# One of four low parts moves from GpSimd to VectorE, with three reorderings around it

## The chip, the cores and the metric

The kernel runs on one core of a Trainium2 chip. A core has TensorE (matrix products), VectorE, ScalarE and GpSimd, each with its own instruction stream, and SyncE, which here only starts DMAs. The streams meet through semaphores. The metric is the device time of one execution in microseconds (us), lower is better.

## The reference, cut to what matters

Three stages: attention masked by hash buckets, a mixture of experts with 8 experts, and a gated two-layer network. The change touches the first.

```
q_bits = (einsum('bhsd,dk->bhsk', q, proj) > 0)      # 6 bits per row, the same for k
mask   = q_bucket[:, :, :, None] == k_bucket[:, :, None, :]
scores = where(mask, scale * (q @ k.T), -1e9)
scores = scores - max(scores, axis=-1)
attn   = exp(scores); attn = attn / (sum(attn) + 1e-9)
out    = attn @ v                                    # 16 heads, 768 rows, width 64
x = moe(out as rows, w_gate, w1, w2)                 # 1536 rows of 512
y = (h * clip(h + 3, 0, 6) / 6) @ w_out,  h = x @ w_in
```

All of it is float32. The kernel multiplies in fp32r, and gets the lost digits back with splits: a tile is rounded to a high part, the low part is tile minus high part, and a product is hi*hi + hi*lo + lo*hi.

## The kernel before, in words

The 768 rows of a head are six chunks of 128 (C = 6). Sixteen heads follow one another in a software pipeline: while the maxima and scores of head h are made, the probability tiles of head h-1 are split and multiplied by v, and q and k of head h+1 are turned, rounded and hashed. The order on each engine is written out by hand, in a function `head` per engine; heads 0 to 2 and the last few are written out, the rest run in loops.

In one head TensorE makes (function names of the code): `max_tile(0)` to `max_tile(5)`, masked scores of a chunk into one of two PSUM tiles, `score_ps`, in turn; `values(0)` to `values(5)`, which is `times_v` of the head before; `turn_qk` and `hash_qk` of the next head into `prep_ps`; then `turn_mean`, `cross(0)`, `turn_max`, `cross(1)`, `turn_back` and the rest of `cross` and `direct`, the final scores. `turn_max` needs `negmax_hl` from VectorE, and the final scores need `turn_max`, since the maximum enters them as two more rows of the product. `turn_max` waits for the semaphore `negmax_ready`.

VectorE splits probability tiles 0 and 1 of the head before (L958, L960), takes the six maxima (L934), between them subtracts the low part of the next q and k (`low_qk`, L923) and makes the hash bits (`bits`, L929), and ends with three small instructions of `minus_max` (L939, L940, L942), the last of which makes `negmax_ready`. ScalarE makes the exponentials (L727), the high parts of tiles 2 to 5 (`high_probs`, L731) and the rounding of the next q and k (`high_qk`, L716). GpSimd makes the low parts of tiles 2 to 5 (`low_probs`, L629), then `low_v` (L624), two instructions of `blend_mean` (L609, L613), three of `sum_v` (L598, L601, L603), and in every other head an eighth of the first expert's low weights (`first_low`, L619).

What waits for what around the change: `hash_qk` waits for `low_qk`; `bits` waits for `hash_qk`; `max_tile(c)` with c of 2 and more waits until maximum c-2 is taken, since it writes the same PSUM tile; `times_v(kc)` waits for the low part of tile kc; a low part waits for its high part. In this text lo(2) to lo(5) are the low parts of tiles 2 to 5, hi(2) to hi(5) the high ones.

Of the kernel before, what the change touches and what calls it, by code (L numbers as in the profile page):

```python
# [19 lines left out]
def hashed_attention_moe_kernel(nc, q, k, v, proj, w_gate, w1, w2, w_in, w_out, out, capacity):  # L20
# [66 lines left out]
    with ctx:  # L87
# [259 lines left out]

        BY_V = 2
        BY_AP = C - BY_V

        setup_steps = [0]
        setup_first, setup_bits = [0], [0]
# [188 lines left out]
        def _(pool):  # L541
# [90 lines left out]
            def head(h, first=False, second=False, last=False, spare=None):  # L632
                if spare:
                    spare()
                if not first:
                    for kc in range(BY_V, C):
                        low_probs(h.prev(), kc)
                low_v(h)
                if not first and not second:
                    blend_mean(h.prev().prev())  # L640
                sum_v(h, first, second)
# [64 lines left out]
        def _(act):  # L706
# [40 lines left out]
            def head(h, first=False, last=False, spare=None):  # L747
                for kc in range(BY_V, C):
                    if not first:
                        high_probs(h.prev(), kc)  # L750
                    if kc == BY_V and not last:
                        high_qk(h.next())
                if spare:
                    spare()
                if not first:
                    copy_out(h.prev())
                copy_max(h, last)
                for c in range(C):
                    exps(h, c, first)
# [127 lines left out]
        def _(dve):  # L887
# [66 lines left out]
            def split_probs(h, count=BY_V):  # L954

                for kc in range(count):
# [3 lines left out]
                    v.tensor_tensor(probs_lo[:, kc, :], probs[:, kc, :], probs_hi[:, kc, :].bitcast(F32),  # L960
                                    ALU.subtract).then_inc(lo_done_v, 1)

            def normalise(h):
                dve.wait_ge(turned_back, h.i + 1)
                dve.wait_ge(f_step, h.i + 1)
                sums = out_ps[0][:, 0:MEAN].rearrange("p (c x) -> p c x", x=XW + 1)
                v.tensor_scalar(denom[:, h.side, :], sums[:, :, XW], EPS, None, ALU.add).then_inc(n_step, 1)
                dve.wait_ge(n_step, h.i * 2 + 1)
                v.reciprocal(recip[:, h.side, :], denom[:, h.side, :]).then_inc(n_step, 1)
                dve.wait_ge(n_step, h.i * 2 + 2)  # L970
                v.tensor_tensor(x_rows[:, :, h.i, :], sums[:, :, 0:XW],
                                recip[:, h.side, :].unsqueeze(2).to_broadcast([P, C, XW]), ALU.mult)
                dve.wait_ge(x_done, h.i + 1)
                v.tensor_copy(mean_sb[:, h.side, :], out_ps[0][:, MEAN:MEAN + XW]).then_inc(out_read, 1)

            def head(h, first=False, second=False, last=False):
# [9 lines left out]
                    low_qk(h.next())  # L986
                take_max(h, 2)
                take_max(h, 3)
                if not last:
                    bits(h.next())  # L990
                take_max(h, 4)
                take_max(h, 5)
                minus_max(h)
                if last:
# [112 lines left out]
            split_probs(LAST, BY_V + 1)  # L1107

            for kc in range(BY_V + 1, C):
                dve.wait_ge(hi_done_a, LAST.i * BY_AP + (kc - BY_V))  # L1110
                v.tensor_tensor(probs_lo[:, kc, :], probs[:, kc, :], probs_hi[:, kc, :].bitcast(F32),
                                ALU.subtract).then_inc(lo_done_v, 1)

            hot_rows(0)
            dve.wait_ge(x_done, HEADS + 1)
# [102 lines left out]
        def _(pe):  # L1218
# [76 lines left out]
            def times_v(h, kc, tail=False):  # L1295


                if kc < BY_V or tail:
                    pe.wait_ge(lo_done_v, h.i * BY_V + (kc + 1))
                else:  # L1300
                    pe.wait_ge(lo_done_p, h.i * BY_AP + (kc - BY_V + 1))
                if kc == 0:
                    pe.wait_ge(v_lo_done, h.i + 1)
                    pe.wait_ge(out_read, h.i + 2)
# [45 lines left out]
            def head(h, first=False, last=False, counted=None):  # L1350
# [13 lines left out]
                prepare(turn_qk, second=first)  # L1364
                values(1)
                max_tile(h, 2, first)
                prepare(hash_qk)
                max_tile(h, 3, first)
                values(2)
                max_tile(h, 4, first)  # L1370
                values(3)
                max_tile(h, 5, first)
# [201 lines left out]
```

## Time and profile before

| | us |
|---|---|
| median of 3 runs | 814.69 (814.51 to 815.03) |
| the profiled execution, its own time | 815.2 |
| its span, first to last instruction | 813.4 |
| attention with routing, up to the first expert product | 0 to 342 |
| experts | 342 to 534 |
| gated network | 534 to 813 |

The span holds 11,427 instructions. The profile gives for each engine the time in which it is busy, and a timeline of instructions with the time for which the engine stood idle ahead of each. TensorE's granted clock was 1.00 of its full 2.4 GHz in the heads that are looked at below. A timeline row that begins before the previous one ends shows overlap at the ends of instructions, or an instruction that has been taken up and is held back.

### The profile page before, as it was taken

To read this page: it belongs to the slowest core of one execution; us is meant where nothing else is said; L and a number is where in the kernel's file an instruction comes from. 1 tells how busy PE (TensorE), PEld (TensorE's weight loads), DVE (VectorE), ACT (ScalarE), POOL (GpSimd) and SP (SyncE) were. 2 spreads that over 40 slices of the span, in tenths; PEclk is the share of its full clock that TensorE was granted. 3 is DMA by queue.
4 is the path that set the end of the run, shared out by engine and by line. 5 is a ranking of instruction groups with operands and counts; after the bars stand their busy time and mean duration, and the time that the engine had idled before them with its cause. 6 is when DMAs were issued, how large, how long until landed. Compare 5 with 4: busy or idle time off the path is not lost.

```text
span 813.4 us, 11427 instructions
## 1 busy us (share of the span) xinstructions
PE 759.0 (93%) x4141; PEld 622.2 (76%) x4141; DVE 445.2 (55%) x703; ACT 357.3 (44%) x543; POOL 233.2 (29%) x225
## 2 busy tenths in 40 slices
PE   3799999999999998499999999949999999999998
PEld 2577777777777766499999999938888888888886
DVE  4577777778788778566555556624343223222222
ACT  2355546565555544066555555523343323232223
POOL 3057676665767674211212210000000000000000
PEclk9899999999999999599999999979999999999999
DMA  5664444444434310746677655371010100010001
GB/s 123 176 190 112 102 103 95 96 116 112 108 96 114 86 25 21 225 166 199 223 242 250 221 188 187 123 248 66 1 36 17 52 1 1 0 52 1 1 0 52
DMA packets 70163, 85.97 MB, mean 106 GB/s; under 512 B 42223, under 2 KB 44271, under 8 KB 69616
## 3 DMA queue, kind: packets, MB, share of 16 engines
q1 hardware_dynamic: 64784, 74.99, 31.8%
q0 software_dynamic: 2560, 7.34, 2.8%
q10 hardware_dynamic: 2784, 3.18, 1.1%
q8 instruction: 21, 0.34, 0.2%
q14 instruction: 14, 0.11, 0.0%
HBM read 58.76 MB, written 13.63 MB: 89 GB/s over the span
## 4 chain that ended last, share of the span: by engine, by line
PE 66%; POOL 14%; issue 10%; DVE 4%; ACT 3%; DMA 2%; POOLq 1%; SPq 0%; ACTq 0%; DVEq 0%
PE score_ps L1439 11%; PE score_ps L1441 11%; PE score_ps L1440 11%; POOL probs_lo L629 8%; PE out_pair L1441 7%; PE out_pair L1439 7%; PE out_pair L1440 7%; PE prep_ps L1428 2%; POOL w_lo L619 1%; PE score_ps L1254 1%; PE out_pair L1307 1%; PE out_pair L1309 1%; PE out_pair L1308 1%; POOL v_lo L624 1%; ACT probs L727 1%
## 5 line engine op out<-in xcount | busy, mean ns | idle before, releaser
L629 POOL TENSOR_TENSOR probs_lo<-probs,probs_hi 128x768 fp32r<-128x768 f32 x60 | 109.5, 1846 | 99.4 <-ACT probs_hi L731 99.4
L1439 PE MATMUL score_ps<-w_hi,h_hi 128*128 128x512 f32 x320 | 126.1, 394 | 0.3 <-DVE h_lo L1203 0.3
L1441 PE MATMUL score_ps<-w_hi,h_lo 128*128 128x512 f32 x320 | 124.7, 390 | 0.0
L1440 PE MATMUL score_ps<-w_lo,h_hi 128*128 128x512 f32 x320 | 124.6, 389 | 0.0
L1196 DVE SCALAR_TENSOR_TENSOR gated<-tclip,out_pair 128x512 f32<-128x512 f32 x48 | 33.0, 688 | 145.3 <-ACT tclip L858 145.3
L1439 PE MATMUL out_pair<-xT_hi,w_hi 128*128 128x512 f32 (+1 forms) x320 | 112.1, 350 | 0.0
L1441 PE MATMUL out_pair<-xT_hi,w_lo 128*128 128x512 f32 (+1 forms) x320 | 110.9, 347 | 0.0
L1440 PE MATMUL out_pair<-xT_lo,w_hi 128*128 128x512 f32 (+1 forms) x320 | 110.9, 347 | 0.0
L934 DVE TENSOR_REDUCE rowmax<-score_ps 128x1 f32<-128x768 f32 x96 | 88.7, 951 | 19.6 <-PE score_ps L1254 19.2
L858 ACT ACTIVATE tclip<-out_pair,three 128x512 f32<-128x512 f32 x48 | 33.1, 690 | 146.5 <-PE out_pair L1441 146.5
L1141 DVE TENSOR_TENSOR w_lo<-w_raw,w_hi 128x1024 fp32r<-128x1024 f32 x72 | 85.9, 1222 | 18.5 <-ACT w_hi L741 18.2
L741 ACT ACTIVATE w_hi<-w_raw 128x1024 fp32r<-128x1024 f32 (+1 forms) x80 | 81.5, 1053 | 0.0
L1439 PEld LDWEIGHTS score_ps<-w_hi,h_hi 128*128 128x128 f32 x320 | 60.1, 188 | 13.1 <-DVE h_lo L1203 1.2
L1441 PEld LDWEIGHTS score_ps<-w_hi,h_lo 128*128 128x128 f32 x320 | 60.0, 188 | 12.7
L1440 PEld LDWEIGHTS score_ps<-w_lo,h_hi 128*128 128x128 f32 x320 | 60.1, 188 | 12.0
L1307 PE MATMUL out_pair<-probs_hi,v_hi 128*65 128x512 f32 x192 | 66.4, 346 | 3.1 <-POOL probs_lo L629 1.7
L1440 PEld LDWEIGHTS out_pair<-xT_lo,w_hi 128*128 128x128 f32 x320 | 60.6, 189 | 7.5
L1441 PEld LDWEIGHTS out_pair<-xT_hi,w_lo 128*128 128x128 f32 x320 | 60.6, 189 | 7.5
L1439 PEld LDWEIGHTS out_pair<-xT_hi,w_hi 128*128 128x128 f32 x320 | 60.5, 189 | 7.4
L1309 PE MATMUL out_pair<-probs_lo,v_hi 128*65 128x512 f32 x192 | 64.8, 337 | 0.0
L1308 PE MATMUL out_pair<-probs_hi,v_lo 128*64 128x512 f32 x192 | 64.6, 336 | 0.0
L727 ACT ACTIVATE probs<-score_ps 128x768 f32<-128x768 f32 x64 | 48.8, 821 | 28.8 <-PE score_ps L1291 28.7
(182 smaller groups left out, 1313.4 us busy)
## 6 DMA issues: line engine op xcount, KB each, us to landing
w_raw<-in_moe_w SPq DMA_DIRECT2D x32, 1024.0 KB, 7.6
w_raw<-in_moe_w_in SPq DMA_DIRECT2D x4, 1024.0 KB, 5.8
w_raw<-in_moe_w_out SPq DMA_DIRECT2D x4, 1024.0 KB, 11.2
qk_raw<-in_q SPq DMA_DIRECT2D x16, 192.0 KB, 3.8
qk_raw<-in_k SPq DMA_DIRECT2D x16, 192.0 KB, 3.9
v_raw<-in_v SPq DMA_DIRECT2D x16, 192.0 KB, 2.5
k_ext<-q_ext SPq DMA_DIRECT2D x16, 192.0 KB, 2.6
k_pair<-q_ext SPq DMA_DIRECT2D x16, 192.0 KB, 3.1
```

The source lines that it names most:

```text
L629: g.tensor_tensor(probs_lo[:, kc, :], probs[:, kc, :], probs_hi[:, kc, :].bitcast(F32), ALU.subtract).then_inc(lo_done_p, 1)
L727: a.activation(probs[:, c, :], exp_ps[c][:, 0:S], ACT.Exp, scale=SCALE).then_inc(exp_done, 1)
L741: a.activation(w_hi[side][:, cols], w_raw[side][:, cols], ACT.Copy).then_inc(whi_done, 1)
L858: a.activation(tclip[:, s % 2, :], g_ps[s % 2], ACT.Relu, bias=three[:, :]).then_inc(g_clip, 1)
L934: v.reduce_max(rowmax[:, h.side, c:c + 1], score_ps[c % 2][:, 0:S], AX.X).then_inc(max_taken, 1)
L1141: return v.tensor_tensor(w_lo[side][:, cols], w_raw[side][:, cols], w_hi[side][:, cols].bitcast(F32), ALU.subtract)
L1307: mm(out_pair[0:D + 1, lo:hi], v_h, probs_hi[:, kc, lo:hi], start=(kc == 0), stop=False)
L1308: mm(out_pair[0:D, lo:hi], v_l, probs_hi[:, kc, lo:hi], start=False, stop=False)
L1309: ins = mm(out_pair[0:D + 1, lo:hi], v_h, probs_lo[:, kc, lo:hi], start=False, stop=(kc == C - 1))
L1439: mm(out_tile, lhs[0], rhs[0], start=first, stop=False)
L1440: mm(out_tile, lhs[0], rhs[1], start=False, stop=False)
L1441: return mm(out_tile, lhs[1], rhs[0], start=False, stop=last)
```

## The change: what it does

The low part of tile 5 is made by VectorE in heads 1 to 15, after the fourth maximum (`take_max(3)`), and no more by GpSimd, which keeps tiles 2, 3 and 4. `bits` goes from ahead of the fifth maximum (`take_max(4)`) to behind it. On TensorE `hash_qk` goes from ahead of `max_tile(3)` to behind `values(2)`. On ScalarE `high_qk` goes from behind hi(2) to behind hi(3). The semaphore counts follow: VectorE now counts three low parts a head, GpSimd three.

```
+        LOW_V, LOW_P = BY_V + 1, BY_AP - 1
 (GpSimd)
-                    for kc in range(BY_V, C):
+                    for kc in range(BY_V, C - 1):
                         low_probs(h.prev(), kc)
 (ScalarE)
-                    if kc == BY_V and not last:
+                    if kc == BY_V + 1 and not last:
                         high_qk(h.next())
 (VectorE)
+            def low_probs(h, kc, tail=False):
+                dve.wait_ge(hi_done_a, h.i * BY_AP + (kc - BY_V + (0 if tail else 1)))
+                v.tensor_tensor(probs_lo[:, kc, :], probs[:, kc, :], probs_hi[:, kc, :].bitcast(F32),
+                                ALU.subtract).then_inc(lo_done_v, 1)
...
                 take_max(h, 3)
+                if not first:
+                    low_probs(h.prev(), C - 1)
+                take_max(h, 4)
                 if not last:
                     bits(h.next())
-                take_max(h, 4)
                 take_max(h, 5)
 (TensorE)
                 if kc < BY_V or tail:
-                    pe.wait_ge(lo_done_v, h.i * BY_V + (kc + 1))
+                    pe.wait_ge(lo_done_v, h.i * LOW_V + (kc + 1))
+                elif kc == C - 1:
+                    pe.wait_ge(lo_done_v, h.i * LOW_V + LOW_V)
                 else:
-                    pe.wait_ge(lo_done_p, h.i * BY_AP + (kc - BY_V + 1))
+                    pe.wait_ge(lo_done_p, h.i * LOW_P + (kc - BY_V + 1))
...
                 max_tile(h, 2, first)
-                prepare(hash_qk)
                 max_tile(h, 3, first)
                 values(2)
+                prepare(hash_qk)
                 max_tile(h, 4, first)
```

VectorE in the loop over the heads, before: from the low part of q and k (`low_qk`) to the end of `minus_max`. REGISTER_ALU and ISA rows are the counts and waits ahead of an instruction; the numbers behind `qk_lo` and `q_ext` are buffer numbers.

```order
L923 TENSOR_TENSOR qk_lo_78<-prep_ps,q_ext_82 128x768
L933 REGISTER_ALU
L934 TENSOR_REDUCE rowmax<-score_ps 128x1
L933 REGISTER_ALU
L934 TENSOR_REDUCE rowmax<-score_ps 128x1
L927 ISA
L928 ISA
L929 TENSOR_SCALAR q_ext_82<-prep_ps,above,weight 64x768
L933 REGISTER_ALU
L934 TENSOR_REDUCE rowmax<-score_ps 128x1
L933 REGISTER_ALU
L934 TENSOR_REDUCE rowmax<-score_ps 128x1
```

VectorE at the same place with the change (all line numbers are one or more higher there).

```order
L935 TENSOR_REDUCE rowmax<-score_ps 128x1
L965 ISA
L966 TENSOR_TENSOR probs_lo<-probs,probs_hi 128x768
L934 REGISTER_ALU
L935 TENSOR_REDUCE rowmax<-score_ps 128x1
L928 ISA
L929 ISA
L930 TENSOR_SCALAR q_ext_82<-prep_ps,above,weight 64x768
L934 REGISTER_ALU
L935 TENSOR_REDUCE rowmax<-score_ps 128x1
```

The low part of tile 5 (L966) stands between the fourth and the fifth maximum, and the bits (L930) now stand behind the fifth.

TensorE in the same loop, before: `max_tile(2)` and what follows it, up to `max_tile(3)`.

```order
L1254 MATMUL score_ps<-k_ext_85,q_ext_83 128x256
L1240 MATMUL prep_ps<-q_ext_82,proj_hi 64x512
L1240 MATMUL prep_ps<-q_ext_82,proj_lo 64x512
L1240 MATMUL prep_ps<-qk_lo_78,proj_hi 64x512
L1240 MATMUL prep_ps<-q_ext_82,proj_hi 64x256
L1240 MATMUL prep_ps<-q_ext_82,proj_lo 64x256
L1240 MATMUL prep_ps<-qk_lo_78,proj_hi 64x256
L1250 REGISTER_ALU
L1254 MATMUL score_ps<-k_ext_85,q_ext_83 128x512
```

TensorE with the change, from the end of `max_tile(2)` over `max_tile(3)` and `values(2)` (L1315 to L1317) to the first product of the hash.

```order
L1260 MATMUL score_ps<-k_ext_85,q_ext_83 128x256
L1256 REGISTER_ALU
L1260 MATMUL score_ps<-k_ext_85,q_ext_83 128x512
L1260 MATMUL score_ps<-k_ext_85,q_ext_83 128x256
L1315 MATMUL out_pair<-probs_hi,v_hi 65x512
L1316 MATMUL out_pair<-probs_hi,v_lo 64x512
L1317 MATMUL out_pair<-probs_lo,v_hi 65x512
L1315 MATMUL out_pair<-probs_hi,v_hi 65x256
L1316 MATMUL out_pair<-probs_hi,v_lo 64x256
L1317 MATMUL out_pair<-probs_lo,v_hi 65x256
L1246 MATMUL prep_ps<-q_ext_82,proj_hi 64x512
```

The six products of the hash stand behind the six products of `values(2)` now, ahead of `max_tile(4)`, where `max_tile(3)` had to wait for them before.

## Rows read from the trace of the kernel before

**Rows 1.** The page, busy time of each engine: us, share of the span, instructions.
```profile
PE 759.0 (93%) x4141; PEld 622.2 (76%) x4141; DVE 445.2 (55%) x703; ACT 357.3 (44%) x543; POOL 233.2 (29%) x225
```

**Rows 2.** Timeline, one loop head, PE: start, duration, line, operation [idle before <- releaser].
```profile
202.22 1.20 PE L1254 MATMUL score_ps<-k_ext,q_ext 96*128 96x512 f32 x4
...
206.00 0.51 PE L1254 MATMUL score_ps<-k_ext,q_ext 96*128 96x512 f32 x2
207.01 0.45 PE L1240 MATMUL prep_ps<-q_ext,proj_hi 128*64 128x512 f32 x1 [0.50 <-DVE qk_lo L923]
...
213.82 0.62 PE L1283 MATMUL score_ps<-qk_lo,k_pair 128*128 128x512 f32 x2
214.36 0.52 PE L1268 MATMUL prep_ps<-identr,negmax_hl 128*2 128x128 f32 x6
...
220.63 1.21 PE L1254 MATMUL score_ps<-k_ext,q_ext 96*128 96x512 f32 x4
```

**Rows 3.** Timeline, the same head, DVE.
```profile
206.00 0.96 DVE L923 TENSOR_TENSOR qk_lo<-prep_ps,q_ext 128x768 fp32r<-128x768 f32 x1 [1.20 <-ACT q_ext L716]
...
208.68 0.96 DVE L934 TENSOR_REDUCE rowmax<-score_ps 128x1 f32<-128x768 f32 x1 [0.86 <-PE score_ps L1254]
209.67 1.07 DVE L929 TENSOR_SCALAR q_ext<-prep_ps,above,weight 64x768 fp32r<-64x768 f32 x1
210.77 1.82 DVE L934 TENSOR_REDUCE rowmax<-score_ps 128x1 f32<-128x768 f32 x2
212.72 0.44 DVE L939 TENSOR_SCALAR negmax<-rowmax 128x6 f32<-128x6 f32 x1
213.08 0.95 DVE L940 TENSOR_SCALAR negmax_hl<-rowmax 128x6 fp32r<-128x6 f32 x1
214.06 0.17 DVE L942 TENSOR_TENSOR negmax_hl<-negmax,negmax_hl 128x6 fp32r<-128x6 f32 x1
```

**Rows 4.** Timeline, the same head, POOL.
```profile
204.26 1.84 POOL L629 TENSOR_TENSOR probs_lo<-probs,probs_hi 128x768 fp32r<-128x768 f32 x1 [6.04 <-ACT probs_hi L731]
206.78 5.46 POOL L629 TENSOR_TENSOR probs_lo<-probs,probs_hi 128x768 fp32r<-128x768 f32 x3 [0.68 <-ACT probs_hi L731]
212.19 0.94 POOL L624 TENSOR_TENSOR v_lo<-v_raw,v_hi 128x384 fp32r<-128x384 f32 x1
213.09 0.91 POOL L609 TENSOR_TENSOR blend<-alone,mean_sb 128x432 f32<-128x432 f32 x1
214.19 1.11 POOL L613 TENSOR_TENSOR x_rows<-x_rows,blend 128x432 f32 x1 [0.19 <-POOL blend L609]
215.26 0.59 POOL L598 TENSOR_TENSOR v_three<-v_raw 128x192 f32<-128x192 f32 x1
215.93 0.32 POOL L601 TENSOR_TENSOR v_two<-v_three 128x64 f32<-128x64 f32 x1
```

**Rows 5.** Timeline, the same head, ACT.
```profile
205.16 0.81 ACT L716 ACTIVATE q_ext<-prep_ps 128x768 fp32r<-128x768 f32 x1 [0.97 <-PE prep_ps L1231]
205.87 2.30 ACT L731 ACTIVATE probs_hi<-probs 128x768 fp32r<-128x768 f32 x3
```

**Rows 6.** Timeline, head 0, DVE and PE.
```profile
24.57 0.96 DVE L934 TENSOR_REDUCE rowmax<-score_ps 128x1 f32<-128x768 f32 x1 [2.05 <-PE score_ps L1254]
...
29.21 0.80 PE L1268 MATMUL prep_ps<-identr,negmax_hl 128*2 128x128 f32 x6 [0.85 <-DVE negmax_hl L942]
```

**Rows 7.** Timeline behind the last head, POOL and DVE.
```profile
311.06 1.22 POOL L609 TENSOR_TENSOR blend<-alone,mean_sb 128x432 f32<-128x432 f32 x1
312.36 1.71 POOL L613 TENSOR_TENSOR x_rows<-x_rows,blend 128x432 f32<-128x432 f32 x1
...
311.55 1.55 DVE L960 TENSOR_TENSOR probs_lo<-probs,probs_hi 128x768 fp32r<-128x768 f32 x1
313.02 1.46 DVE L958 CAST probs_hi<-probs 128x768 fp32r<-128x768 f32 x1
```

**Rows 8.** One line's instructions: count, then duration in ns, least/median/most.
```profile
L960 DVE TENSOR_TENSOR probs_lo<-probs,probs_hi x33: 957/958/1548, 33.4 to 316.0; 128x768 fp32r<-128x768 f32 x33
```

More of the change, by code:

```diff
@@ L1109, in _ @@
             for kc in range(BY_V + 1, C):
-                dve.wait_ge(hi_done_a, LAST.i * BY_AP + (kc - BY_V))
-                v.tensor_tensor(probs_lo[:, kc, :], probs[:, kc, :], probs_hi[:, kc, :].bitcast(F32),
-                                ALU.subtract).then_inc(lo_done_v, 1)
+                low_probs(LAST, kc, tail=True)
             hot_rows(0)
```

## The prediction

> **What bounds the kernel now.** I read the busy times first: TensorE is busy for 93% of the span [rows 1], so the question is not which engine is full but where TensorE stands still in the one stage that the change touches, the 16 heads. Then the timeline of one head in the loop, engine by engine. A head lasts from 202.22 to 220.63, 18.41 us [rows 2]; all starts below are of this head. The reader is to see two places on TensorE. At 206.00 comes max_tile(2), and the hash behind it starts only at 207.01, with 0.50 us of idle time that ends with VectorE's low_qk [rows 2]. And turn_max starts at 214.36, 0.13 after the third small instruction of minus_max ends (214.06 + 0.17 = 214.23) [rows 2, 3]. From turn_max on everything follows: final scores, exponentials, the next head. So turn_max is where the head's length is decided, and VectorE's minus_max is what it waits for last; TensorE itself was at cross(0) from 213.82, and is hardly ahead.
>
> Then VectorE from low_qk (206.00) to 214.23 [rows 3]. Two things lengthen it. It idles 0.86 us before its fourth maximum (208.68), because max_tile(3) stands behind the hash. And its small instructions take 0.44 and 0.95 us where the third takes 0.17. Both ends agree with GpSimd's: L939 ends at 213.16, low_v at 212.19 + 0.94 = 213.13; L940 ends at 214.03, blend at 213.09 + 0.91 = 214.00 [rows 3, 4]. VectorE is held until the GpSimd instruction in progress is over.
>
> **Does the new instruction meet the same hold?** It is a subtraction of two SBUF tiles, L960's kind. That takes 0.957 us at the least and 1.548 at the most [rows 8]. The long one is at 311.55, and runs into GpSimd's blend, which began at 311.06 and took 1.22 to 312.28; it ends at 313.10, 0.82 after that. GpSimd's next instruction, at 312.36, then takes 1.71 where its like takes 1.11 in the loop [rows 4, 7]. So a two-tile subtraction on VectorE and a GpSimd instruction run one after the other, in the order in which they come, and VectorE loses 0.14 of its 0.96 less. The Trainium skill has two rules on this. "Advanced Engine Details and Errata", Mode Summary, names only GpSimd and VectorE's two-port modes as blocking each other, and by it the subtraction, one element per cycle, would go free; that is rival A below. "SBUF — State Buffer", "SBUF: two separate sides", adds VectorE operations with two SBUF inputs against a GpSimd operation that reads SBUF, held for the whole instruction. The row at 311.55 sides with the second.
>
> **The change part by part, in a loop head.**
>
> ScalarE: rounding waits 0.97 for TensorE's turned q and k [rows 5]; hi(3) takes 2.30 / 3 = 0.77 and fits in this gap. Cost nothing, cover left 0.2. hi(4) and hi(5) end when they did.
>
> GpSimd: lo(2) starts at 204.26 as before. lo(3) no longer waits 0.68, and one low part is gone: three at 5.46 / 3 = 1.82 each end at 204.26 + 5.46 = 209.72, where four ended at 206.78 + 5.46 = 212.24 [rows 4]. No new wait comes of this on TensorE: lo(3) and lo(4) end 0.7 to 0.8 earlier than now (208.6 and 210.4 now, by the same spacing), and values(3) and values(4) come at most 0.65 earlier.
>
> TensorE: max_tile(3) and values(2) fill the hash's gap. What it saves is the 0.50 idle, up to 0.65 with the start of the pair before it; lo(2) is done in time (204.26 + 1.84 = 206.10). values(5) finds its low part at 210.54, where it now comes at 212.24. So TensorE arrives at turn_max 0.5 to 0.65 earlier. That is the most that a head can gain.
>
> VectorE: low_qk ends at 206.96, two maxima (1.82 for two [rows 3]) end near 208.7, the idle 0.86 is gone. The low part of tile 5 arrives at 208.7, while GpSimd is in lo(4) until 209.72. Held for 1.0; it ends 0.82 after, 210.54. Then the fifth maximum 0.91 (211.4), bits 1.10 (start to start, 209.67 to 210.77; 212.5), the sixth maximum to 213.5, and L939 after 0.13 (as 210.77 + 1.82 = 212.59 to 212.72 now): 213.6, 0.9 later than now. What is queued behind the held instruction is exactly this chain, and turn_max behind it.
>
> Now the small ones. GpSimd's low_v is held by the new low part until 210.54 and ends near 211.35, blend near 212.2, the x_rows addition (starts 1.10 after blend, takes 1.11) near 213.5, v_three 0.59 to 214.1, v_two 214.15 to 214.45 [rows 4]. L939 at 213.6 falls into v_three and ends near 214.1, L940 fits in ahead of v_two (214.2), L942 either fits in as well or ends with v_two: 214.3 to 214.5, against 214.23. The 0.9 is bought back for the most part, because the holds by low_v and blend (0.27 and 0.78) become one of about 0.35. A head is 0.07 to 0.27 longer. I take 0.15, below the middle, because turn_back waits for ScalarE's copy, which moves up with the earlier mean. Bounds for one head: -0.65 (TensorE takes over as the limit) and +0.65 (each small instruction one GpSimd instruction later).
>
> **Sum.** Thirteen heads of this kind (2 to 14): 13 x 0.15 = +1.95. Head 1 has no blend and x_rows: +0.1. Head 0 makes no low part of tile 5, but its fourth maximum waits 2.05 for the hash, and turn_max 0.85 for negmax_hl [rows 6]; with the hash later the fourth maximum is out of the way during it, and the 0.85 goes: -0.85. Head 15 has no next head; TensorE is fed there by GpSimd's low parts, tile 4 is held up by VectorE's tile 5, and their sum stays: 0. Behind the last head GpSimd's leftovers hold L960 by 0.59 and L958 by about 0.9 [rows 7, 8]; GpSimd comes 0.8 earlier there, its additions move from the second split to the first, and of 1.5 lost about half comes back: -0.7, bounds 0 and -1.5. Everything behind it (routing, gathers, experts, the gated network) is untouched and shifts along. Together 1.95 + 0.1 - 0.85 - 0.7 = +0.5 on the profiled execution's 815.2, 815.7. That execution is 0.5 above the median of the runs, 814.69, so the median forecast is 815.2.
>
> **Rivals.**
> A, the new low part isn't held (its place in the loop differs from the tail's). It ends at 209.6, L939 comes at 212.65, GpSimd's additions are over by then up to a part of x_rows or v_three, negmax_hl is ready near 213.5, and turn_max is limited by TensorE: -0.65 x 13 - 1.45 = -9.9, 804.8. For it: low_qk (one SBUF tile) keeps its 0.96 beside GpSimd. Against: the 1.55 us row.
> B, a hold that pays more than it gives back: slower. At 213.6 VectorE's three small instructions stand before v_three, v_two and v_sum, one behind the other. If L940 comes behind v_two and L942 behind v_sum, negmax_hl is ready near 214.9, +0.65 a head: 8.5 + 0.1 - 1.55 = +7, 821.7. It decides where L940 comes 0.13 us later than I work out. For it: in the present trace two of three are caught. Against: v_two and v_sum are short, with gaps between them.
> C, the chain arrives 0.15 us earlier, L939 goes in ahead of v_three, and one hold is left: negmax_hl at 214.1, -0.1 a head, -1.3 - 1.45 = -2.8, 811.9.
> D, the change does what it says and nothing moves: TensorE's rest only goes from the hash to turn_max, and the terms of head 0 and the tail are eaten by the loop. This is my forecast's mechanism with other small terms, 814.7.
>
> **How the numbers follow.** Forecast with D 0.57 (own range 812.9 to 818), A 0.12, B 0.16, C 0.15. A measurement of this kernel tells 0.2% from no change, 1.6 us: 813.1 to 816.3. The forecast case gives about 0.38 of same, 0.04 of faster, 0.15 of slower. Faster 0.12 + 0.15 + 0.04 = 0.31, slower 0.16 + 0.15 = 0.31, same 0.38. The range takes in C and B and leaves out A: 808 to 822.
>
> **What would show it.** In a loop head after: the idle time before the hash gone; the new VectorE subtraction 1.8 to 1.9 us long, ending 0.82 after lo(4), and low_v stretched to about 1.7; the idle before the fourth maximum gone; idle before turn_max on TensorE grown to 0.6 to 0.9, with negmax_hl as releaser; heads of 18.5 to 18.7. A subtraction of 0.96 in all heads, and heads under 18, would make A true and this forecast wrong; L940 or L942 of 0.3 and more each, with heads near 19, B. Head 0's turn_max should come 0.85 earlier in any case.

## The result, and the profile after

| | us |
|---|---|
| before, median of 5 runs beside the changed kernel | 815.03 (814.51 to 817.27) |
| after, median of 5 runs | 827.39 (823.71 to 835.46) |
| ratio | 1.0163, 95% interval 1.0111 to 1.0216 |
| profiled execution after, its span, its mean granted clock | 835.46, 833.3, 0.963 (before 0.977) |

The change makes the kernel slower, by 12.4 us at the median, where the forecast was 815.2. Not only the time has grown, its spread has too: the five runs of after lie 12 us apart, those of before 3. The profiled execution is the slowest of the five.

The page of after, busy time of each engine, against [rows 1]:

```profile
PE 770.0 (92%) x4141; PEld 636.0 (76%) x4141; DVE 456.0 (55%) x718; ACT 359.2 (43%) x543; POOL 215.4 (26%) x210
```

Fifteen low parts have moved from GpSimd to VectorE (225 to 210 and 703 to 718 instructions). TensorE does the same 4141 instructions and is busy 11 us longer: its instructions themselves have become longer. That is the first sign of a slower clock, and it isn't the profiled execution alone: the mean granted clock over a whole execution is 0.959 to 0.969 in the five runs of after, and 0.977 to 0.981 in every run of before beside the experiments below.

I measure a head from one turn_max to the next. Before, the first of the 15 heads takes 19.17 us and the others 18.33 to 18.53 (18.43 is typical). After, in the profiled execution, the lengths from turn_max(0) on are 19.80, 19.78, 21.38, 21.67, 22.96, 18.66, 19.89, 18.67, 22.75, 20.09, 18.66, 18.67, 18.59, 18.73 and 18.46. Heads of three sorts are among them. (Head h runs from the turn_max of head h-1 to its own, so head 3 begins at 67.88.) The windows of five of these heads, with the columns start:end, length, busy time of each engine, granted clock, DMA share and GB/s:

```profile
67.88:89.26 21.38, 20.31 (x106) 16.22 (x107) 14.60 (x22) 10.26 (x14) 12.60 (x11) 0.84 0.39 91
89.26:110.93 21.67, 17.88 (x106) 13.63 (x107) 17.33 (x22) 10.83 (x15) 12.66 (x11) 1.00 0.43 104
110.93:133.89 22.96, 21.95 (x106) 17.71 (x107) 14.61 (x22) 10.27 (x14) 10.00 (x9) 0.78 0.30 71
133.89:152.55 18.66, 17.68 (x106) 13.68 (x107) 14.30 (x22) 10.80 (x15) 10.23 (x10) 1.00 0.44 104
191.11:213.86 22.75, 20.59 (x106) 16.16 (x107) 15.99 (x22) 10.27 (x14) 12.63 (x11) 0.85 0.36 85
```

The head from 133.89 is undisturbed. The heads from 67.88 and 110.93 have TensorE busy for 20.3 and 22.0 us with the same 106 instructions, at a mean granted clock of 0.84 and 0.78. The head from 89.26 has the full clock and the same TensorE time as an undisturbed one (17.88), but VectorE is busy for 17.33 us instead of 14.3. The head from 191.11 has both.

**An undisturbed head.** DVE, POOL and PE up to turn_max at 191.11, which answer to [rows 2 to 4] (L940, L941 and L943 are L939, L940 and L942, L630 is L629, L1274 is L1268):

```profile
185.09 1.97 DVE L966 TENSOR_TENSOR probs_lo<-probs,probs_hi 128x768 fp32r<-128x768 f32 x1
...
190.14 0.45 DVE L940 TENSOR_SCALAR negmax<-rowmax 128x6 f32<-128x6 f32 x1
190.50 0.16 DVE L941 TENSOR_SCALAR negmax_hl<-rowmax 128x6 fp32r<-128x6 f32 x1
190.69 0.28 DVE L943 TENSOR_TENSOR negmax_hl<-negmax,negmax_hl 128x6 fp32r<-128x6 f32 x1
...
182.55 3.69 POOL L630 TENSOR_TENSOR probs_lo<-probs,probs_hi 128x768 fp32r<-128x768 f32 x2
186.15 1.70 POOL L625 TENSOR_TENSOR v_lo<-v_raw,v_hi 128x384 fp32r<-128x384 f32 x1
187.81 0.91 POOL L610 TENSOR_TENSOR blend<-alone,mean_sb 128x432 f32<-128x432 f32 x1
...
191.11 0.52 PE L1274 MATMUL prep_ps<-identr,negmax_hl 128*2 128x128 f32 x6 [0.92 <-DVE negmax_hl L943]
```

The new subtraction takes 1.97 us, held by GpSimd's second of the two low parts, which ends at 186.24; low_v behind it is held in turn and takes 1.70 where it took 0.94 in [rows 4]. L940 is caught by v_three, the other two are nearly free. TensorE is through with cross(0) and stands still for 0.92 us ahead of turn_max, where it stood still for nothing in [rows 2]. The head is 0.23 us longer than before (18.66 against 18.43).

**What follows the rest.** The final scores behind turn_max at 191.11, on PE:

```profile
194.14 1.65 PE L1297 MATMUL score_ps<-q_ext,k_ext 98*128 98x512 f32 x4
195.58 0.84 PE L1289 MATMUL prep_ps<-qk_lo,k_pair 128*128 128x512 f32 x2
...
199.92 0.52 PE L1297 MATMUL prep_ps<-q_ext,k_ext 98*128 98x512 f32 x2
```

A pair takes 0.84 at 195.58 and 0.52 again at 199.92. Between, TensorE works at 1.2 in place of 2.4 GHz. What TensorE did before each head, the idle time ahead of turn_max, in the profiled execution of after (start of turn_max, rest, granted clock below 1.00 in the head that it begins, if any):

| | 67.88 | 89.26 | 110.93 | 133.89 | 152.55 | 172.44 | 191.11 | 213.86 | 233.95 | 252.61 |
|---|---|---|---|---|---|---|---|---|---|---|
| rest | 1.29 | 1.07 | 2.99 | 1.00 | 0.91 | 0.90 | 0.92 | 1.44 | 1.17 | 0.89 |
| clock | 0.84 | | 0.78 | | 0.91 | | 0.85 | 0.92 | | |

Before, all these rests are 0, and the rest that the change removes ahead of the hash was 0.50. After, the three longest are each followed by a fall, and of the seven from 0.89 to 1.17 two are; the three rests behind the table's end, of 0.91, 0.78 and 0.99, are not. The 2.99 and the 1.44 end the two heads with a long hold.

**The second sort: a long hold.** VectorE's new subtraction and GpSimd in the same head:

```profile
206.33 3.86 DVE L966 TENSOR_TENSOR probs_lo<-probs,probs_hi 128x768 fp32r<-128x768 f32 x1
...
202.10 5.51 POOL L630 TENSOR_TENSOR probs_lo<-probs,probs_hi 128x768 fp32r<-128x768 f32 x3 [8.27 <-ACT probs_hi L732]
207.55 0.95 POOL L625 TENSOR_TENSOR v_lo<-v_raw,v_hi 128x384 fp32r<-128x384 f32 x1
208.44 0.93 POOL L610 TENSOR_TENSOR blend<-alone,mean_sb 128x432 f32<-128x432 f32 x1
```

The subtraction stands at VectorE's head from 206.33. GpSimd's low part ends at 207.61; but then low_v goes, unstretched, and blend too. The subtraction ends at 210.19, 0.82 after the end of blend (208.44 + 0.93 = 209.37). Two GpSimd instructions have passed it, and it waited for three. The other long one is at 101.90 and takes 3.82, some 1.9 more than usual. In its head the chain, late by that much, then meets one more hold: the first small instruction waits for the end of GpSimd's w_lo (108.17 + 2.34 = 110.51) and takes 1.73 where it takes 0.45 above. The two together make the rest of 2.99:

```profile
108.80 1.73 DVE L940 TENSOR_SCALAR negmax<-rowmax 128x6 f32<-128x6 f32 x1
...
108.17 2.34 POOL L620 TENSOR_TENSOR w_lo<-w_raw,w_hi  x1
```

**Head 2.** The loads of w_raw that SP issues behind the move of bits, and ScalarE, of after:

```profile
47.13 1.18 SPq L438 DMA_DIRECT2D w_raw<-in_moe_w  x2
...
56.73 1.58 ACT L732 ACTIVATE probs_hi<-probs 128x768 fp32r<-128x768 f32 x2 [1.13 <-DMA w_raw<-in_moe_w]
```

and of before:

```profile
45.78 1.20 SPq L437 DMA_DIRECT2D w_raw<-in_moe_w  x2
```

bits comes later on VectorE, SP issues the loads behind it 1.35 later, and ScalarE waits for the loads.

**Where the 20.3 us of the profiled execution went** (835.46 against 815.2; each number is the sum of differences of head lengths):

| | us |
|---|---|
| turn_max of head 0 | -0.91 |
| heads 1 and 2 (loads, slow clock at the start) | +1.88 |
| heads of a low clock alone (from 67.88, 110.93, 152.55, 213.86) | +10.62 |
| head of a long hold and of the hold by w_lo (from 89.26) | +3.23 |
| head of a long hold and a low clock (from 191.11) | +4.32 |
| six undisturbed heads and head 15 | +1.44 |
| from the last turn_max to the end | -0.68 |
| outside the span | +0.4 |

An undisturbed head is 0.23 longer too, and the long hold at 206.33 is 1.89 longer than the usual one. Without these parts the low clock accounts for 10.62 - 4 x 0.23 + 4.32 - 0.23 - 1.89 = 11.9, some 12 us of the 20.3. This is the slowest of the five runs; no profile shows how the 12.4 us of the median divide.

### The profile page after: what moved, and what is told of

Read it like the earlier page. It is cut to its first block, busy times and chain, and to the rows that moved or that the text cites. A ratio compares the mean times of both kernels' runs of the same rounds, so it can differ in the third digit from the quotient of the medians.

```text
span 833.3 us, 11381 instructions
## 1 busy us (share of the span) xinstructions
PE 770.0 (92%) x4141; PEld 636.0 (76%) x4141; DVE 456.0 (55%) x718; ACT 359.2 (43%) x543; POOL 215.4 (26%) x210
## 4 chain that ended last, share of the span: by engine, by line
PE 74%; DVE 12%; issue 5%; ACT 3%; DMA 3%; POOL 1%; SPq 0%; DVEq 0%; POOLq 0%; ACTq 0%
PE score_ps L1447 11%; PE score_ps L1449 10%; PE score_ps L1448 10%; PE out_pair L1447 7%; PE out_pair L1448 7%; PE out_pair L1449 7%; DVE rowmax L935 5%; PE score_ps L1297 3%; PE out_pair L1339 3%; PE score_ps L1260 2%; PE score_ps L1289 2%; DVE q_ext L930 2%; PE prep_ps L1436 2%; ACT probs L728 2%; PE out_pair L1315 1%
## 5 line engine op out<-in xcount | busy, mean ns | idle before, releaser
L630 POOL TENSOR_TENSOR probs_lo<-probs,probs_hi 128x768 fp32r<-128x768 f32 x45 | 83.0, 1877 | 136.3 <-ACT probs_hi L732 136.3
L1147 DVE TENSOR_TENSOR w_lo<-w_raw,w_hi 128x1024 fp32r<-128x1024 f32 x72 | 85.9, 1222 | 18.5 <-ACT w_hi L742 18.3
L1315 PE MATMUL out_pair<-probs_hi,v_hi 128*65 128x512 f32 x192 | 66.2, 345 | 4.7 <-POOL probs_lo L630 2.4
L1317 PE MATMUL out_pair<-probs_lo,v_hi 128*65 128x512 f32 x192 | 64.7, 337 | 0.0
## 6 DMA issues: line engine op xcount, KB each, us to landing
w_raw<-in_moe_w_out SPq DMA_DIRECT2D x4, 1024.0 KB, 11.9
```

What stands on the lines that cost most here:

```text
L630: g.tensor_tensor(probs_lo[:, kc, :], probs[:, kc, :], probs_hi[:, kc, :].bitcast(F32), ALU.subtract).then_inc(lo_done_p, 1)
L1147: return v.tensor_tensor(w_lo[side][:, cols], w_raw[side][:, cols], w_hi[side][:, cols].bitcast(F32), ALU.subtract)
L1315: mm(out_pair[0:D + 1, lo:hi], v_h, probs_hi[:, kc, lo:hi], start=(kc == 0), stop=False)
L1317: ins = mm(out_pair[0:D + 1, lo:hi], v_h, probs_lo[:, kc, lo:hi], start=False, stop=(kc == C - 1))
```

## The experiments

### One part at a time

Theory at this point: the reorderings and the move are two changes of opposite sign. e1_reorder_only is before with the three reorderings alone (all four low parts stay on GpSimd):

```
@@ before: ScalarE, high_probs            @@ VectorE
-  if kc == BY_V and not last:               +  take_max(h, 4)
+  if kc == BY_V + 1 and not last:               bits(h.next())
      high_qk(h.next())                      -  take_max(h, 4)
@@ TensorE
-  prepare(hash_qk)
   max_tile(h, 3, first)
   values(2)
+  prepare(hash_qk)
```

> The three reorderings alone; GpSimd makes all four low parts again. Theory T (the price is VectorE's new subtraction, which waits for GpSimd instructions in progress): without it VectorE's chain ends near 213.55 where it ended at 214.23 in a head of before, so a head takes about 17.75 to 17.9 and not 18.43, TensorE's clock stays at full speed, and the time is 804 to 808. Rival U (the later hash or the later rounding is what costs, through bits, the moves that wait for them and the loads behind these): 820 or more, as with the change.

e2_move_only is the changed kernel with these same edits taken back, so that the move of the low part is alone.

> Only the low part of tile 5 moves to VectorE, behind the fourth maximum; hash, rounding and bits stand where they stood before. Theory T: VectorE keeps its idle time ahead of the fourth maximum and gets the held subtraction (1.6 to 2.0 us) as well, negmax_hl comes 0.7 to 0.9 later than before in each of 14 heads, 11 us, and TensorE's clock falls in some heads on top: 826 to 842. Rival U: 813 to 818, since nothing is reordered.

Measured: e1 808.67 (805.88 to 809.81), ratio 0.9915 [0.9896, 0.9933], its median 0.7 above the expected range and its typical head inside its own; e2 838.55 (833.19 to 839.79), ratio 1.0263 [1.0230, 1.0296], as expected.

| head, undisturbed | order before | order changed |
|---|---|---|
| last low part on GpSimd | 18.43 | 17.79 |
| last low part on VectorE | 19.36 | 18.66 |

In undisturbed heads the two are additive: the reorderings give 0.64 to 0.70 a head, the move costs 0.87 to 0.93. e1 beats both kernels. Its VectorE and TensorE ahead of turn_max:

```profile
200.32 0.96 DVE L923 TENSOR_TENSOR qk_lo<-prep_ps,q_ext 128x768 fp32r<-128x768 f32 x1 [1.22 <-ACT q_ext L716]
...
206.86 0.80 DVE L939 TENSOR_SCALAR negmax<-rowmax 128x6 f32<-128x6 f32 x1
207.77 0.17 DVE L942 TENSOR_TENSOR negmax_hl<-negmax,negmax_hl 128x6 fp32r<-128x6 f32 x1
...
207.47 0.62 PE L1283 MATMUL score_ps<-qk_lo,k_pair 128*128 128x512 f32 x2
208.07 0.52 PE L1268 MATMUL prep_ps<-identr,negmax_hl 128*2 128x128 f32 x6
```

VectorE now needs 7.62 us from low_qk to the end of the third small instruction (200.32 to 207.94), where it needed 8.23 [rows 3], and TensorE has lost its 0.50 ahead of the hash. Both chains have become shorter by about 0.6, and TensorE still runs through cross(0) into turn_max with no rest. The windows of one head of e1 and of an undisturbed and a disturbed one of e2:

```profile
190.28:208.07 17.79, 17.71 (x108) 13.65 (x108) 13.21 (x21) 10.77 (x16) 11.37 (x11) 1.00 0.46 109
```

```profile
87.38:109.34 21.96, 20.55 (x106) 16.12 (x107) 14.34 (x22) 11.32 (x15) 10.29 (x10) 0.84 0.38 88
109.34:128.70 19.36, 17.95 (x107) 13.62 (x107) 14.13 (x22) 9.82 (x14) 12.62 (x11) 1.00 0.42 100
```

In e1 TensorE is busy for 17.71 of 17.79. In e2 it rests for 1.4 us in a head (19.36 less 17.95), and heads of a clock of 0.84 and 0.92 come back, though its subtraction is never held for long:

```profile
L966 DVE TENSOR_TENSOR probs_lo<-probs,probs_hi x18: 949/1706/2041, 43.5 to 340.2; 128x768 fp32r<-128x768 f32 x18
```

So the low clock doesn't need the long hold.

### The long hold

e3_low_v_waits lets GpSimd's low_v wait until VectorE's low part is made, so that nothing can pass it:

```
@@ after: GpSimd
+  if not first:
+      pool.wait_ge(lo_done_v, h.prev().i * LOW_V + LOW_V)
   low_v(h)
```

> The change, and GpSimd's low_v waits until VectorE has made the low part of tile 5. Theory T, its part on the long holds (3.8 us in 2 of 15 heads, where low_v and blend went ahead of the waiting subtraction): none is above 2.3 us now, these heads lose their extra 1.9 us and the clock drop behind it, 4 to 9 us of the profiled execution, and the runs spread less: 816 to 824. Rival: the long holds have another cause (VectorE itself), they stay, and the time stays at 823 to 835.

Measured: 824.04 (820.54 to 824.81), 1.0090 [1.0070, 1.0110], at the upper end of what was expected. The subtraction in all its instances (count, least/median/most ns), of after and of e3:

```profile
L966 DVE TENSOR_TENSOR probs_lo<-probs,probs_hi x18: 951/1971/3861, 42.3 to 338.7; 128x768 fp32r<-128x768 f32 x18
```

```profile
L968 DVE TENSOR_TENSOR probs_lo<-probs,probs_hi x18: 950/1959/2298, 41.0 to 326.2; 128x768 fp32r<-128x768 f32 x18
```

The long holds are gone, undisturbed heads are as long as ever (18.50 to 18.63), and the low clock stays, in four heads; the first:

```profile
66.67:87.96 21.29, 20.31 (x107) 16.23 (x107) 14.60 (x23) 10.26 (x14) 11.71 (x11) 0.84 0.39 91
```

Long holds and low clock are two mechanisms.

### The low clock

e4_fill gives TensorE two more mean products, into a sum that the next product overwrites, between cross(0) and turn_max; the result doesn't change:

```
@@ after: TensorE, ahead of the product of the mean
+  if not first and not last:
+      pe.wait_ge(v_summed, h.prev().i + 1)
+      for _ in range(2):
+          mm(mean_T_ps, v_sum[:, h.prev().side, :], mean_w[:, :], start=True, stop=True)
```

> The change, and TensorE repeats the small mean product twice more ahead of turn_mean (about 0.36 us each), in the time in which it would stand still before turn_max. Results are the same. Theory T, its part on the clock (after a stand of 0.9 us and more TensorE's granted clock falls to half for some us): the clock stays full in the heads but for those with a long hold, final scores take 0.35 and not 0.64 us a pair, and the time is 815 to 822. Rival (the clock falls for another reason, or the stand is not what triggers it): as the change, 823 to 835, plus up to 0.2 us a head for the added products.

Measured: 821.81 (819.74 to 825.80), 1.0076 [1.0052, 1.0100]. The products are shorter than I had put down: the rest ahead of turn_max is 0.38 to 0.57 in ten of 13 heads where it was 0.9. In the profiled execution heads 3 to 14 take 18.62 to 18.73 at a clock of 1.00, but for two neighbours. The windows of these two:

```profile
179.98:200.02 20.04, 18.42 (x111) 14.10 (x111) 15.68 (x22) 9.81 (x14) 12.61 (x11) 1.00 0.41 97
200.02:220.13 20.11, 19.39 (x110) 15.37 (x111) 14.71 (x22) 11.13 (x15) 10.01 (x9) 0.92 0.41 96
```

The first has a hold of 3.73 us at 192.62, and TensorE rests for 1.00 at its end; the clock falls in the head behind it, and only there. With the rest shortened by 0.4 in most heads one fall is left where the profile of after has five, and it follows the longest rest but that of head 0.

e11_rest_only makes the same rest without the subtraction: e1 with the sixth maximum taken a second time, into a scrap tile. e12_rest_filled is e11 with four more mean products in the rest.

```
@@ e1 to e11: VectorE, ahead of take_max(h, 5)    @@ e11 to e12: TensorE, as in e4
+  if not first:                                  +  for _ in range(4):
+      dve.wait_ge(max_scores, h.i * C + 6)       +      mm(mean_T_ps, ...)
+      v.reduce_max(scrap[:, 1:2], score_ps[1][:, 0:S], AX.X)
```

> The three reorderings alone (a head of 17.78 us, no clock fall in the heads), and VectorE takes the sixth maximum a second time into an unused place, 0.95 us more ahead of minus_max in heads 1 to 15. GpSimd's work is as before, only TensorE's rest ahead of turn_max grows, to 0.8 us or a little more. Theory T (the rest is what lets the clock fall): heads of 18.5 to 18.7 us with the clock full, and some of 19.8 to 21.5 with it fallen to half for a part; 818 to 832, with a wide spread of the runs. Rival (the falls of the changed kernel come from something else, the held subtraction or GpSimd): every head 18.5 to 18.7 us, clock full, 819 to 821, runs within 2 us.

> As the one before, and TensorE makes four more of the small mean products (some 0.6 us in all) in the rest. Theory T: the same length of head from VectorE, but no clock fall: 818 to 821 and runs within 3 us. Rival: as the one before without these products, fallen heads among them.

Measured: e11 820.22 (819.75 to 824.82), 1.0075 [1.0052, 1.0098]; e12 823.08 (820.11 to 823.85), 1.0097 [1.0078, 1.0116]. Two windows of e11:

```profile
103.14:123.14 20.00, 18.99 (x106) 14.94 (x107) 14.31 (x23) 10.10 (x14) 13.70 (x12) 0.91 0.41 97
123.14:141.94 18.80, 17.74 (x106) 13.64 (x107) 14.23 (x23) 10.79 (x15) 11.34 (x11) 1.00 0.44 103
```

A rest alone, with no held subtraction in the program, is followed by a low clock once in e11, and e1, which differs from it by one maximum, has none. In e11 the rests are 0.87 to 1.02, and the fall is behind one of 0.98, one of twelve alike. The median of e11 would fit the rival too. What decides is the clock: 0.975 in four of the six runs, and 0.967 and 0.969 in the two slowest, 822.75 and 824.82. In e12 there is no rest, no head falls (18.74 to 18.89), and the mean clock is 0.975 to 0.981 in all four runs. So filling the rest keeps the clock up, but it saves no time here, and e12's 818 to 821 was missed: three of its runs take 3 us more than the profiled one. No trace shows where.

The same count for all kernels but e5, e6 and e8. The rests are those ahead of the turn_max that begin heads 3 to 15, a fall is a granted clock below 1.00 in such a head, both in the profiled execution, and the last column has the mean granted clock of every whole run:

| | rests | heads of 13 with a fall | mean clock of the runs |
|---|---|---|---|
| before, e1 | 0 | 0 | 0.977 to 0.981 |
| e12 | 0 | 0 | 0.975 to 0.981 |
| e10 | 0 to 0.50 | 0 | 0.975 to 0.979 |
| e7 | 0.39 to 0.53 | 1, behind 0.49 | 0.973 to 0.979 |
| e4 | 0.38 to 0.57, 0.72, 0.82, 1.00 | 1, behind 1.00 | 0.971 to 0.975 |
| e11 | 0, twelve of 0.87 to 1.02 | 1 | 0.967 to 0.975 |
| e3 | 0.71 to 1.32 | 4 | 0.967 to 0.973 |
| e9 | 0, 0.81 to 1.25 | 2 | 0.963 to 0.973 |
| after | 0.78 to 2.99 | 5 | 0.959 to 0.969 |
| e2 | 0.76 to 0.94 | 6 | 0.961 to 0.965 |

No head of these falls behind a turn_max without a rest, and by and large the clock of the runs is lower where there is more rest. But no length divides the two: e7 has a fall behind a rest of 0.49, and e9 has none behind one of 1.25. (In e5, e6 and e8, below, turn_max has no rest ahead of it, or one of 0.16. Only head 12 of e5 falls, with a rest of 2.60 in its middle.) The rest and the fall of e7:

```profile
176.45 0.52 PE L1274 MATMUL prep_ps<-identr,negmax_hl 128*2 128x128 f32 x6 [0.49 <-DVE negmax_hl L943]
```

```profile
176.45:195.94 19.49, 19.00 (x106) 14.89 (x107) 14.11 (x22) 10.07 (x14) 12.61 (x11) 0.91 0.42 99
```

### The loads of head 2, and all three cures together

e9_loads_ahead lets SP issue the loads of w_raw ahead of the move of bits in heads 1 and 2. e10_three is the changed kernel with the edits of e3, e4 and e9.

```
@@ after: SP, place_head
+  if ahead:
+      ahead()          # heads 1 and 2: the first loads, which stood behind place_head
```

> The change, and SyncE issues the first expert's four weight loads ahead of the move of the hash bits in heads 1 and 2, not behind it. Theory T (the later bits hold back these loads on SyncE's queue, and ScalarE waits 1.13 us for the weights in head 2): this wait goes, 1.1 us once, 826 where the change has 827, not to be told apart in the median but seen in the trace. Rival (the wait is for bandwidth, not for the issue): it stays.

> The change with three cures at once: low_v waits for the low part of tile 5, two more mean products in TensorE's rest, and the weight loads ahead of the move of the bits. Theory T (long holds, clock falls and the load are all that there is on top of the 0.2 us a head that I had forecast): all heads from 3 on take 18.55 to 18.75 us with the clock full, 816.5 to 819.5, and the runs spread by less than 2 us. Rival (an unknown part is left): over 820 or spread as the change.

Measured: e9 823.46 (820.67 to 833.53), 1.0116 [1.0073, 1.0160]. ScalarE's wait is gone, and head 2 takes 18.54 instead of 19.78:

```profile
53.76 1.62 ACT L735 ACTIVATE probs_hi<-probs 128x768 fp32r<-128x768 f32 x2
```

Two later heads still fall (21.54 and 20.10), and the runs lie 13 us apart, as the changed kernel's do: the three with a mean clock of 0.971 to 0.973 take 820.67 to 821.16, the three with 0.963 to 0.965 take 825.77 to 833.53. e10: 817.99 (816.29 to 819.91), 1.0032 [1.0021, 1.0044]. Its heads 3 to 14 take 18.52 to 18.68, at the full clock, like this one:

```profile
102.99:121.58 18.59, 18.23 (x110) 14.12 (x111) 14.22 (x22) 9.72 (x14) 11.95 (x11) 1.00 0.45 104
```

Its rests are 0.27 to 0.50 from there on. From after to e10 the ratio falls from 1.0163 to 1.0032, or from 13.3 us over before to 2.6: four fifths of the loss are the three mechanisms. What stays is about the forecast's own term: heads 3 to 14 are 0.13 to 0.33 longer than before's. The spread is 3.6 us, more than the 2 that I expected and far less than 12.

### Was it GpSimd's small holds?

The forecast counted the holds of L939 and L940 [rows 3] as time that could be bought back. e6_before_and_wait is before, with GpSimd's low_v waiting until negmax is ready, so that no hold is possible. e5_reorder_and_wait has the same wait on top of e1.

```
@@ GpSimd
+  if not first:
+      pool.wait_ge(negmax_ready, h.i + 1)
   low_v(h)
```

> The kernel before, and low_v waits until negmax_hl is ready: the holds of L939 and L940 (0.27 and 0.78 us a head) go. Theory T (in the kernel before TensorE itself arrives only 0.1 us ahead of negmax_hl, since its rest is at the hash): 813 to 815.5, 0.1 us a head. Rival (the holds set the length of a head): a head is 0.7 to 1.0 us shorter, 801 to 806.

> The three reorderings alone (all low parts on GpSimd), and GpSimd's low_v waits until negmax_hl is ready, so that nothing holds VectorE's three small instructions. Theory T: L939 takes 0.17 and not 0.8 us, negmax_hl is ready 0.4 us or more before TensorE wants it, turn_max follows cross(0) without a rest, a head takes 17.6 to 17.75 us and not 17.78: 806 to 809, at most 2 us less than with the reorderings alone. Rival: low_v and what follows it come 0.8 us later and something else on the path waits for them (v_sum, the next v load, x_rows): over 810.

Measured: e6 821.43 (820.78 to 822.11), 1.0083 [1.0068, 1.0098]; e5 823.08 (821.41 to 826.01), 1.0102 [1.0084, 1.0120]. Both expected times were missed, and e6 fits its rival no better; e5's rival, over 810 since something waits for GpSimd's later work, came true. The small instructions do take 0.17 each in both. But in e6 the heads take 18.45 and 18.92 in turn, with one of 20.94: without the hold the head isn't shorter, since TensorE arrives at turn_max at the same time [rows 2]. And GpSimd's work comes later by the same amount. In e5, where heads 5, 7, 9, 11 and 13 take about 20.15, head 12 takes 23.42 at a clock of 0.93, and the others of the loop about 17.8, GpSimd and VectorE show where it goes:

```profile
180.18 2.42 POOL L619 TENSOR_TENSOR w_lo<-w_raw,w_hi  x1
184.57 6.19 POOL L629 TENSOR_TENSOR probs_lo<-probs,probs_hi 128x768 fp32r<-128x768 f32 x3 [1.98 <-ACT probs_hi L733]
...
180.41 2.40 DVE L954 CAST v_hi<-v_raw 128x384 fp32r<-128x384 f32 x1
184.78 2.48 DVE L962 TENSOR_TENSOR probs_lo<-probs,probs_hi 128x768 fp32r<-128x768 f32 x1
```

w_lo now lies over the copy v_hi, which is held for 2 us in place of 0.35, and the low part of tile 1 meets GpSimd's first. TensorE waits for low parts of VectorE in such a head, twice, for 0.66 and 1.00 us. A hold that was ordered away in one place came back in another and cost more.

### The place and the source of the subtraction

e7_low_earlier puts VectorE's low part one maximum earlier (ahead of the fourth instead of the fifth). e8_low_from_psum leaves it there and reads a tile of scores in PSUM instead of probs.

```
@@ after: VectorE, e7                  @@ e8, in place of low_probs
-  take_max(h, 3)                      +  v.tensor_tensor(probs_lo[:, C - 1, :], score_ps[1][:, 0:S],
   if not first:                       +                  probs_hi[:, C - 1, :].bitcast(F32),
       low_probs(h.prev(), C - 1)      +                  ALU.subtract).then_inc(lo_done_v, 1)
+  take_max(h, 3)
```

> The change, with VectorE's low part of tile 5 one place earlier, ahead of the fourth maximum and not behind it. Two SBUF inputs. Theory T (it goes through only when no GpSimd instruction is in progress): it arrives at the boundary of GpSimd's lo(3) and lo(4), so it takes either 1.0 to 1.3 us or, behind lo(4), 2.6 to 2.9 us; 812 to 832 by which it is. Rival (no lock, a fixed price of place): as the change, 1.95.

> As the one before (ahead of the fourth maximum), but the subtraction reads the scores of the fourth maximum in PSUM in the place of the probability tile, so that only one input is in SBUF; the low part of tile 5 is left out of the result. Theory T (two SBUF inputs are what is held): 0.96 us in all heads beside GpSimd's low parts, negmax_hl earlier, a head of 17.7 to 18.0 us: 803 to 810. Rival (any VectorE instruction that writes or reads SBUF beside GpSimd's is held at this place): 1.9 us or more, and no less time than the one before.

Measured: e7 815.46 (813.57 to 818.71), 1.0004 [0.9992, 1.0017], heads of 18.21 to 18.47 but for the first two and the one of 19.49 with the low clock shown above. e8's total can't be compared (1279.16: its result is wrong, other work runs behind the attention stage, and TensorE makes 5133 instructions in place of 4141), but its heads can: 17.63 to 17.77. The subtraction in each:

```profile
L966 DVE TENSOR_TENSOR probs_lo<-probs,probs_hi x18: 951/1012/2299, 41.4 to 318.0; 128x768 fp32r<-128x768 f32 x18
```

```profile
L997 DVE TENSOR_TENSOR probs_lo<-score_ps,probs_hi x15: 948/948/958, 41.3 to 289.2; 128x768 fp32r<-128x768 f32 x15
```

and GpSimd's three low parts beside it, of e7 and of e8:

```profile
204.25 6.23 POOL L630 TENSOR_TENSOR probs_lo<-probs,probs_hi 128x768 fp32r<-128x768 f32 x3 [7.66 <-ACT probs_hi L732]
```

```profile
197.71 5.49 POOL L630 TENSOR_TENSOR probs_lo<-probs,probs_hi 128x768 fp32r<-128x768 f32 x3 [7.79 <-ACT probs_hi L732]
```

In e7 VectorE's subtraction falls into a gap between two of GpSimd's and goes at once; GpSimd loses 0.74 instead. In e8 neither loses anything. So most of the price of the move, 0.9 a head, hangs on the place and the source of the subtraction: over e1's 17.79 a head costs about 0.5 in e7 and nothing in e8. The hold is paid by whichever engine comes second, or, with one operand in PSUM, by neither. As e8 reads other data, it shows the price of an instruction and no kernel that could be used.

## Why the prediction was wrong

Right, step by step:

- The hold. "Held for 1.0; it ends 0.82 after": it takes 1.97, low_v stretches to 1.70 (forecast 1.7). The Trainium skill, "SBUF — State Buffer", "SBUF: two separate sides", says this of two SBUF inputs against a GpSimd operation that reads SBUF, and the trace agrees; e8's 0.948 with one PSUM operand agrees too. Rival A, a free subtraction, was wrong where the change puts it.
- The idle time before the hash and before the fourth maximum is gone, and TensorE's rest is ahead of turn_max (forecast 0.6 to 0.9, measured 0.92). An undisturbed head is 18.66 (forecast 18.5 to 18.7, +0.23 against the 0.15 chosen).
- The small instructions: L940 (L939 before) runs into v_three, the other two are nearly free, as worked out. Rival B's catches by v_two and v_sum didn't occur; in one head w_lo caught L940 for 1.73, which no rival had.
- The tail: -0.68 (forecast -0.7), of which 0.51 comes by the last of the splits behind the last turn_max, where the forecast had put it. ScalarE's rounding in its gap cost nothing.

Wrong:

- **The step that failed is "TensorE's rest only goes from the hash to turn_max", with nothing charged behind it.** (The words are rival D's, which the forecast calls its own mechanism.) It expected the rest there "grown to 0.6 to 0.9", and it was 0.92, but counted its length alone; what the clock does after it was a term put at nothing without a reason. In the profiled execution five heads follow with a granted clock between 0.78 and 0.92, worth some 12 of the 20 us. [Rows 2] show a rest of 0.50 at another place, ahead of the hash, that the full clock survives in every head; they don't show what one ahead of turn_max does, and the forecast had no rival for it. e1 (no rest, no fall), e11 (the same kernel with a rest: a fall, and a lower clock in its two slowest runs) and e12 (the rest filled: none) name the cause; e3 shows that it needs no long hold, and e4 and e10 that shorter rests bring fewer falls.
- **"One after the other, in the order in which they come"** was read off one row [rows 7]. In 2 of 15 heads GpSimd's next two instructions go ahead of VectorE's that waits: 3.8 us in place of 1.9 or 2. e3 shows that order on GpSimd removes it.
- **SP's queue was not priced.** bits later by one maximum and a held subtraction moves the loads behind it by 1.35 us, and ScalarE waits 1.13 in head 2. e9 removes it.
- **Head 0's number was luck.** turn_max came 0.91 earlier, and the forecast had 0.85, but not by the step it gave. TensorE's rest ahead of turn_max, which was to go, is 1.70 where it was 0.85: TensorE arrives earlier still. The gain is VectorE's, whose wait ahead of the fourth maximum falls from 2.05 [rows 6] to 1.18. And of the 0.91 only 0.27 stays. The clock of TensorE reaches its full value in both kernels only at about 35 us, so that the earlier start is spent on slow pairs. PE of after and then of before, down to the next head's first max_tile:

```profile
34.63 0.84 PE L1297 MATMUL score_ps<-q_ext,k_ext 98*128 98x512 f32 x2
35.91 0.52 PE L1297 MATMUL prep_ps<-q_ext,k_ext 98*128 98x512 f32 x2
36.27 0.86 PE L1260 MATMUL score_ps<-k_ext,q_ext 96*128 96x512 f32 x4
```

```profile
34.27 0.84 PE L1291 MATMUL score_ps<-q_ext,k_ext 98*128 98x512 f32 x2
35.48 0.51 PE L1291 MATMUL score_ps<-q_ext,k_ext 98*128 98x512 f32 x2
36.54 0.96 PE L1254 MATMUL score_ps<-k_ext,q_ext 96*128 96x512 f32 x4
```

- The forecast saw that 0.65 was the most a head could gain, and that the move costs about 0.9. It never asked what the reorderings bring without the move, which is the better kernel.

Open: why a rest ahead of turn_max, of 0.5 as of 1.2 us, is followed by a low clock in some heads and not in others, so also which runs come out at 824 and which at 835; whether its place among small products matters (e5 has rests of 1.0 between the products of values, and the five heads with one keep the full clock); and what decides in which heads GpSimd passes the waiting VectorE. No run here tells any of these.

## What to carry to other kernels

Where two engines arrive at a meeting point together, work moved onto one of them costs its full length, and the other's rest at that point has to be priced beyond its length: a rest at a place where the trace of before has none is an unknown cost, and the range has to reach to the slow side for it. Split a change into reordering and moving before judging it: here one part gains 7 us and the other loses some 20. And here a wait on a semaphore ordered the hold between VectorE and GpSimd and did not remove it (e3, e5, e6); an operand in PSUM removed it (e8).

## What the runs showed of the hardware that was not expected

- TensorE is busy for 17.68 of 18.66 us in an undisturbed head, and still its rests ahead of turn_max are followed, in some heads, by work at half the clock: pairs of 0.84 in place of 0.52, a head longer by 1.2 to 4.3 us. Mostly the rests are of 0.8 us and more; one is of 0.49 (e7).
- A VectorE instruction that waits for one of GpSimd's can be passed by GpSimd's next two: 3.82 and 3.86 us, twice in 15 heads, and 3.73 once in e4.
- The same fp32 subtraction of 128x768 takes 0.948 us with a PSUM operand beside GpSimd's low parts, and GpSimd's three take 5.49; with two SBUF operands either it is held (1.97) or GpSimd is (6.23 for three).
- Instructions of six elements a row are held as well: L940 took 1.73 at 108.80 in the changed kernel, up to the end of GpSimd's w_lo.
